# Second MLP of a three-part kernel: second product in float32r parts, low parts on GpSimd, no magnitude before the sine, another order

## The reference

```
def _moe2_ref(x, w_in, w_out) -> np.ndarray:
    h = x @ w_in
    g = h * np.cos(h)
    return (g @ w_out).astype(np.float32)
...
    attn_out = _attn_ref(**attn_kwargs)
    x = attn_out.reshape(B * S, D)
    x = _moe_ref(x=x, **moe_kwargs)
    return _moe2_ref(x=x, **moe2_kwargs)
```

## Time and profile before

| | |
|---|---|
| median of 3 runs | 2904.14 us (2903.19 to 2906.07) |
| the profiled execution, device time | 2907.74 us |
| span of the profiled execution, first to last instruction | 2905.8 us |
| PE busy | 2819.3 us (97%) |
| DVE busy | 2591.5 us (89%) |
| ACT busy | 2510.5 us (86%) |
| POOL busy | 1408.3 us (48%) |

### The profile page before, as it was taken

The page is one execution under the profiler, slowest core; times in us unless marked ns, Lnnn a source line. Parts: engine busy times, 40 slices in busy tenths (PEclk is TensorE's granted clock), DMA queues, the critical chain, the costliest instruction groups (busy, mean ns, idle before and its releaser), DMA issues.

```text
span 2905.8 us, 38889 instructions
## 1 busy us (share of the span) xinstructions
PE 2819.3 (97%) x10159; PEld 1702.5 (59%) x10159; DVE 2591.5 (89%) x3357; ACT 2510.5 (86%) x3341; POOL 1408.3 (48%) x841
## 2 busy tenths in 40 slices
PE   8969999999999999999999899999999999999999
PEld 5535555555555555555555466666666666666665
DVE  4559999999999999999999899999999999999998
ACT  4449999999999999999999788888888888888887
POOL 0019999999999999999999600000000000000000
PEclk9979999999999999999999999999999999999999
DMA  4200000000002000000000000000000000000000
GB/s 121 82 14 11 7 10 10 7 10 10 7 10 68 11 10 7 10 7 10 10 7 7 1 7 11 11 10 11 11 13 10 11 10 11 10 11 10 11 10 14
DMA packets 25713, 45.68 MB, mean 16 GB/s; under 512 B 2888, under 2 KB 11880, under 8 KB 25384
## 3 DMA queue, kind: packets, MB, share of 16 engines
q1 hardware_dynamic: 25640, 44.92, 5.1%
HBM read 16.99 MB, written 12.78 MB: 10 GB/s over the span
## 4 chain that ended last, share of the span: by engine, by line
PE 50%; POOL 32%; issue 10%; ACT 4%; DVE 3%; POOLq 1%; DMA 0%; ACTq 0%; DVEq 0%; SPq 0%
PE bank L816 24%; POOL work L304 18%; PE bank L905 18%; POOL work L302 13%; PE bank L760 2%; PE bank L740 2%; PE bank L809 1%; ACT work L380 1%; ACT work L372 1%; PE bank L733 1%; DVE work L630 1%; PE bank L896 1%; ACT work L383 1%; PE bank L750 1%; POOLq L300 1%
## 5 line engine op out<-in xcount | busy, mean ns | idle before, releaser
L816 PE MATMUL bank<-work,v 128*128 128x480 f32 x3328 | 1486.5, 569 | 21.3 <-ACT tokens_t L389 20.8
L816 PEld LDWEIGHTS bank<-work,v 128*128 128x128 f32 x3328 | 618.1, 189 | 438.6 <-issue 386.0
L809 PE MATMUL bank<-part_hi,stack_now 96*128 96x480 f32 x2496 | 695.0, 405 | 24.8 <-DVE work L630 4.5
L809 PEld LDWEIGHTS bank<-part_hi,stack_now 96*128 96x128 f32 x2496 | 424.5, 189 | 386.4 <-DVE work L630 272.1
L304 POOL TENSOR_TENSOR work<-work 128x960 f32<-128x960 f32 x278 | 625.8, 2251 | 23.2
L692 DVE SCALAR_TENSOR_TENSOR work<-work,bank 128x960 f32<-128x960 int32 x416 | 479.7, 1153 | 83.4 <-ACT work L441 81.2
L612 DVE SCALAR_TENSOR_TENSOR bank<-bank,coef_a,work 128x960 f32<-128x960 f32 x416 | 506.3, 1217 | 16.9 <-PE bank L809 13.0
L630 DVE SCALAR_TENSOR_TENSOR work<-bank,coef_a,work 128x960 f32<-128x960 f32 x416 | 502.7, 1208 | 1.6
L367 ACT ACTIVATE work<-work 128x960 f32<-128x960 f32 x416 | 418.7, 1006 | 78.9 <-POOL work L304 69.1
L701 DVE TENSOR_TENSOR work<-work,bank 128x960 f32<-128x960 f32 x416 | 476.9, 1146 | 0.3 <-ACT work L446 0.3
L905 PE MATMUL bank<-part_hi,w_hi 128*128 128x480 f32 x832 | 467.6, 562 | 4.3 <-DVE work L701 2.7
(11 more groups left out here) (81 smaller groups left out, 2005.4 us busy)
## 6 DMA issues: line engine op xcount, KB each, us to landing
x_ring<-in_x_dram SPq DMA_DIRECT2D x52, 240.0 KB, 2.9
x_group<-tokens_t SPq DMA_DIRECT2D x52, 240.0 KB, 2.2
out_dram<-work SPq DMA_DIRECT2D x52, 240.0 KB, 2.4
stack_now<-stack_next SPq DMA_DIRECT2D x8, 288.0 KB, 3.0
work<-in_moe_w_in_dram SPq DMA_DIRECT2D x1, 1024.0 KB, 10.0
w_raw<-in_moe_w_in_dram SPq DMA_DIRECT2D x1, 1024.0 KB, 5.1
v<-in_moe_w_out_dram SPq DMA_DIRECT2D x2, 0.5 KB, 10.7
ind<-in_inducing_dram SPq DMA_DIRECT2D x1, 16.0 KB, 1.8
```

What stands on the lines that cost most here:

```text
L809: mm = pe.matmul(place_out[:, t, :], stack_now[:, i, w], part_hi[0:K3, place, :], start=start, stop=stop, skip_group_check=not start)
L816: mm = pe.matmul(sums, v[:, 2 * u + t, :], g[:, t * GROUP:(t + 1) * GROUP], start=(2 * u + t == 0), stop=(2 * u + t == CHUNKS - 1))
```

## The change

The hidden values are now split at 0.25 turns off: L495 adds 0.25 before the rounding, so the remainder h - 2 pi turns lies in a range on which sine of (remainder + pi/2) can be taken directly. Both magnitude instructions (L433, L696) are gone. The product h cos(h) is written in place, into `angle`, which has four buffers instead of three, and `act2` is gone.

Three of four chunks of the second product go in float32r parts, with three matmuls each (`parts_out`, L968): ScalarE copies the product into a high part `act2_hi` (L508), GpSimd subtracts it to make the low part `act2_lo` (L361). An even unit has both of its chunks in parts (960 columns, **wide** below), an odd unit only the first (480 columns, **narrow**); its second chunk stays a float32 matmul. The weights `v2` are split by GpSimd in four pieces before the first product. The parts lie where `stack_now` was.

GpSimd also splits each group's tokens (`high_y` L344, `low_y` L349). The two output copies move from ScalarE to VectorE (L729, L735). TensorE's step k is now `end2(k)`, `begin2(k + 5)`, and a due `turn_out`; ScalarE's is L495 of unit k+4, L499 of k+3, L508 of k+2; VectorE's L749 of k+4 and L755 of k+3; GpSimd's L361 of k+2. L749 of unit n waits for `end2` of unit n-4, L508 of unit n for `end2` of unit n-2. The diff, cut to its core:

```diff
-PART_Y, KEEP_OUT_T, TURN_OUT, KEEP_OUT = -5, 11, 10, 13
+HID2, TURN2, SINE, HIGH, LOW = 5, 4, 3, 2, 2
+PART_Y, KEEP_OUT_T, TURN_OUT, KEEP_OUT = -9, 9, 11, 12
...
+        v2_hi = at(stack_at, "v2_hi", [P, CHUNKS, C], F32R)
+        act2_hi = at(stack_at + 4 * F, "act2_hi", [P, 2, UNIT], F32R)
+        act2_lo = at(stack_at + 4 * F + 8 * UNIT, "act2_lo", [P, 2, UNIT], F32R)
...
-        angle = [cut(2), cut(3), cut(4)]
-        act2 = [cut(5), cut(6), cut(7)]
+        angle = [cut(2), cut(3), cut(4), cut(5)]
...
+            def low_part(n0, k):
+                n, w = n0 + k, slice(0, split_to(k))
+                pool.wait_ge(act2_hi_ready, n + 1)
+                nc.gpsimd.tensor_tensor(act2_lo[:, k % 2, w], angle[k % 4][:, w], act2_hi[:, k % 2, w].bitcast(F32),
+                                        ALU.subtract).then_inc(act2_parted, 1)
+            def units2(n0, ks):
+                for k in ks:
+                    g = group_due(k, PART_Y)
+                    new = g is not None and exists(n0 // GROUP_UNITS + g)
+                    if new:
+                        high_y(n0 // GROUP_UNITS + g, y_place(g))
+                        pool.wait_ge(y_hi_ready, n0 // GROUP_UNITS + g + 1)
+                    if k + LOW >= 0 and exists_unit(n0 + (k + LOW)):
+                        low_part(n0, k + LOW)
+                    if new:
+                        low_y(n0 // GROUP_UNITS + g, y_place(g))
+            high_y(0, y_place(0))
+            pool.wait_ge(y_hi_ready, 1)
+            low_y(0, y_place(0))
+            pool.wait_ge(v2_loaded, 16)
+            pool.wait_ge(hid_ready, UNITS)
+            for j in range(CHUNKS // 4):
+                part_v2(j)
...
-                    nc.scalar.activation(q[:, SPLIT:], q[:, SPLIT:], ACT.Abs).then_inc(act_folded, 1)
...
-                    nc.scalar.activation(halves(turns[k % 2]), buf(k), ACT.Identity, scale=1.0 / (2 * pi)).then_inc(turns_ready, 1)
...
-                    nc.scalar.activation(q, q, ACT.Sin, scale=-1.0, bias=pi / 2).then_inc(cos_ready, 1)
...
+                    nc.scalar.activation(halves(turns[j % 2]), buf(j), ACT.Identity, scale=1.0 / (2 * pi), bias=0.25).then_inc(turns_ready, 1)
+                if k + SINE >= 0 and exists_unit(n0 + (k + SINE)):
+                    n, q = n0 + (k + SINE), angle[(k + SINE) % 4]
+                    act_.wait_ge(angle_ready, n + 1)
+                    nc.scalar.activation(q, q, ACT.Sin, bias=pi / 2).then_inc(cos_ready, 1)
+                if k + HIGH >= 0 and exists_unit(n0 + (k + HIGH)):
+                    n, j, w = n0 + (k + HIGH), k + HIGH, slice(0, split_to(k + HIGH))
+                    act_.wait_ge(act2_ready, n + 1)
+                    if not isinstance(n, int) or n >= 2:
+                        act_.wait_ge(act2_used, n - 1)
...
+                    nc.scalar.copy(act2_hi[:, j % 2, w], angle[j % 4][:, w]).then_inc(act2_hi_ready, 1)
...
-                    if later or n >= 3:
-                        dve.wait_ge(act2_ready, n - 2)
+                    if not isinstance(n, int) or n >= 4:
+                        dve.wait_ge(act2_used, n - 3)
...
+                    q = halves(angle[j % 4])
+                    dve.wait_ge(cos_ready, n + 1)
+                    nc.vector.tensor_tensor(q, q, buf(j), ALU.mult).then_inc(act2_ready, 1)
...
+                    if (t + 1) * GROUP <= split_to(k):
+                        pairs = ((v2_hi, act2_hi[:, b, w]), (v2_hi, act2_lo[:, b, w]), (v2_lo, act2_hi[:, b, w]))
+                    else:
+                        pairs = ((v2, angle[k % 4][:, w]),)
...
-                pe.wait_ge(act2_ready, n + 1)
+                pe.wait_ge(act2_parted, n + 1)
...
-                    if exists_unit(n0 + (k + LEAD)):
-                        begin2(n0, k + LEAD)
+                    if k >= 0 and exists_unit(n0 + k):
+                        end2(n0, k)
+                    if k + HID2 >= 0 and exists_unit(n0 + (k + HID2)):
+                        begin2(n0, k + HID2)
```

More of the change, by code:

```diff
@@ L316, in _, with high_y @@
             units(LAST, range(1, UNITS - LAST))
+            def high_y(g, place):
+                y = tokens_t[:, bass.ds(g * GROUP, GROUP)]
+                later = not isinstance(g, int)
+                if later or g >= PLACES:
+                    pool.wait_ge(hid2_ready, (g - PLACES + 1) * GROUP_UNITS)
+                else:
+                    pool.wait_ge(num_ready, UNITS - (PLACES - 1 - g) * GROUP_UNITS)
+                    pool.wait_ge(y_kept, g + 1)
+                nc.gpsimd.tensor_copy(part_hi[:, place, :], y).then_inc(y_hi_ready, 1)
@@ new lines, in _ @@
+            high_y(0, y_place(0))
[5 more added lines that the diff above has]
+                part_v2(j)
+            units2(0, range(PART_Y + 1, PEEL))
+            with pool.Fori(0, LOOPS // 2) as i:
+                n0 = pool.snap(i * 2 * BODY)
+                units2(n0, range(PEEL, 2 * BODY + PEEL))
+            units2(LAST, range(PEEL, UNITS - LAST))
@@ new lines, in keep_out @@
+            def keep_out(g, place):
+                dve.wait_ge(out_turned, g + 1)
+                if not isinstance(g, int) or g >= 1:
+                    dve.wait_ge(out_written, g * 16)
+                nc.vector.tensor_copy(out_sb, place[0:SUB, :]).then_inc(out_ready, 1)
+            def unit2(n0, k):
+                g = group_due(k, KEEP_OUT)
+                if g is not None and exists(n0 // GROUP_UNITS + g):
+                    keep_out(n0 // GROUP_UNITS + g, out_bank(g))
+                if k + TURN2 >= 0 and exists_unit(n0 + (k + TURN2)):
+                    n, j = n0 + (k + TURN2), k + TURN2
@@ L704, in units2 @@
                 for k in ks:
[L705 to L709 removed]
+                    unit2(n0, k)
             unit(LAST, UNITS - LAST - 1)
[L712 removed]
             keep_last_y()
             dve.wait_ge(act_ready, UNITS)
[L715 removed]
@@ L716, in _ @@
-            units2(0, range(1, PEEL))
+            units2(0, range(-TURN2, PEEL))
             with dve.Fori(0, LOOPS // 2) as i:
@@ L906, in product_in, with parts_out @@
                 return mm
+            def parts_out(sums, k):
+                u, b = k % GROUP_UNITS, k % 2
+                for t in range(2):
+                    c, w = 2 * u + t, slice(t * GROUP, (t + 1) * GROUP)
+                    if (t + 1) * GROUP <= split_to(k):
+                        pairs = ((v2_hi, act2_hi[:, b, w]), (v2_hi, act2_lo[:, b, w]), (v2_lo, act2_hi[:, b, w]))
+                    else:
+                        pairs = ((v2, angle[k % 4][:, w]),)
+                    for i, (lhs, rhs) in enumerate(pairs):
+                        mm = pe.matmul(sums, lhs[:, c, :], rhs, start=(c == 0 and i == 0), stop=(c == CHUNKS - 1 and i == len(pairs) - 1))
+                return mm
             def begin2(n0, k):
@@ L940, in steps2 @@
                         turn_out(n0 // GROUP_UNITS + g, out_bank(g))
-                    if k >= 0 and exists_unit(n0 + k):
-                        end2(n0, k)
-            steps2(0, range(-3, -2))
+            steps2(0, range(-HID2, -HID2 + 1))
             steps(LAST, range(UNITS - LAST - 2, UNITS - LAST - 1))
-            steps2(0, range(-2, -1))
+            steps2(0, range(-HID2 + 1, -HID2 + 2))
             steps(LAST, range(UNITS - LAST - 1, UNITS - LAST))
-            steps2(0, range(-1, PEEL))
+            steps2(0, range(-HID2 + 2, PEEL))
             with pe.Fori(0, LOOPS // 2) as i:
```

105 lines of the change are left out of this document (40 added, 65 removed).

## The result

The changed kernel takes **2819.5 us** (median of 4 runs, 2816.08 to 2820.59) against 2903.66 for the kernel before, run beside it (4 runs, 2903.05 to 2906.07): a ratio of 0.9707, with a 95% interval of 0.969 to 0.9723. The forecast was 2830, in a range of 2808 to 2865. The sign and the source of the gain were right. The sum is 10.5 us too high, and mostly in the very wait on which it spent most of its working. One of the ten executions of experiment 1 took 3952.67 us, at a granted clock of 0.65 where the others have 0.99, and is left out of its median.

The account below looks back on a forecast made before the run. The prediction took TensorE to bound the second MLP: 2905.8 span - 92.0 (product in parts) + 16.6 (new wait) - 1.9 (join) + 3.5 (end) = 2832.0 span, hence 2830 us median, range 2808 to 2865.

Parts of the forecast that it names:

- The product in parts: TensorE's second product: 12 of 16 chunks save 0.148 us each, 1.77 a group, -92.0 us in 52 groups.
- cost nothing by load: Second MLP: the work moved onto ScalarE, VectorE and GpSimd fits inside TensorE's group time of 22.0 us, adding nothing.
- The low part at 2.25: GpSimd's wide subtraction takes 2.25 us, the median of L304, between bounds of 1.14 and 2.53; a narrow one 1.15.
- held up: Rival: GpSimd's wide low part takes 2.53 us, the chain is 0.44 late, 2859 us; chance 0.17.
- in need of a second pass: Rival: GpSimd needs a rounding pass too, a wide low part costs 3.40 us, 2949 us, slower than before; chance 0.12.
- The new wait: Wide `end2` waits for its low part: chain 5.52 against TensorE's window 5.36, two of four stall, 0.32 a group, +16.6 us.
- the rival in which TensorE alone sets the pace: Rival: the chain through GpSimd is 0.16 or more shorter than forecast, nothing stalls, 2813 us; chance 0.20.
- the forecast's own case: Parts save TensorE time, less some stalls for the low part: 2818 to 2848 us; chance 0.48.
- Join and end: Start of the second MLP -1.9 us (token parts earlier, `begin2` of unit 3 at 1665.2); last `end2` units' waits +3.5 us.
- VectorE's margin of 0.1: From `end2`'s end VectorE's angle and product take 2.5 us against TensorE's 2.61 or more: holds by 0.1, no cost.
- The token work's 0.1 to spare: GpSimd's token copy and subtraction (1.75 us) end at about 8.5, the next high part is ready at 8.6: no cost.
- No loss by the shared ports: GpSimd beside VectorE in the second MLP: every VectorE instruction has a PSUM operand, so neither delays the other, loss nothing.

Follow-up runs that it names:

- experiment 1: The changed kernel with the second product back in plain float32 matmuls, the parts still made but unread: 2904.18 us, ratio 1.0003 to the kernel before.
- experiment 2: The changed kernel with TensorE waiting for the low part only after all matmuls that don't read it: 2816.65 us, ratio 0.9702.
- experiment 3: The changed kernel with each wide low part made in two GpSimd instructions of 480 columns: 2827.86 us, ratio 0.974.
- experiment 4: The changed kernel with each wide low part made in four GpSimd instructions of 240 columns: 2856.73 us, ratio 0.984.
- experiment 7: The changed kernel with the narrow units' high part made by VectorE instead of ScalarE, on its own semaphore: 2881.99 us, ratio 0.9913.
- experiment 9: The changed kernel with a second, long satisfied wait (for the product) ahead of GpSimd's low part: 2819.54 us, ratio 0.971.
- experiment 11: The changed kernel with the token parts of groups 1 and on made by VectorE instead of GpSimd: 2831.48 us, ratio 0.9753.
- experiment 10: All chunks in parts, low part used last, six angle buffers (2808.7 us), with token parts of groups 1 and on moved to VectorE: 2910.06 us, ratio 1.0025.
- experiment 5: The changed kernel with all 16 chunks of the second product in parts, so every unit is wide: 2861.77 us, ratio 0.9842.
- experiment 12: All chunks in parts, low part used last, six angle buffers (2808.7 us), with GpSimd's token work spread over three gaps: 2779.78 us, ratio 0.9579.

## Why the prediction was right, and where its sum was off

**The product in parts, -92.0 us: right.** The six matmuls start 0.22 apart (2213.29, 2213.51). Without stalls the period should have been 23.78 - 1.77 = 22.01; the change has 22.07 and experiment 2, without the wait, 22.03. Experiment 1 gives it all back.

**ScalarE, VectorE, GpSimd "cost nothing by load": right.** They are busy for 987, 921 and 765 of 1080 us. The copies took 0.65 to 0.68 for 0.66 and 0.70, the high part 0.98 for 1.00. Experiment 1 shows that what they were relieved of was worth nothing beside the old product.

**The low part at 2.25: right** (2.26, at most 2.28), and so GpSimd was neither held up nor in need of a second pass. The narrow one took 1.23, for 1.15: an instruction has a fixed share, which experiments 3 and 4 show, too (four of 240 columns take 2.69).

**The new wait, +16.6 us: the step that failed.** The window, the order of the chain and how close it is held, and so did the number of units that pay. Which of them pay did not: in experiment 4 a stall didn't spare the next wide unit, because of the token work. One borrowed term was too large, the 0.26 until GpSimd starts. It was read from L302 in the first MLP and taken for a price of waiting on another engine. Measured are 0.08 behind ScalarE, 0.09 behind VectorE (experiment 7), 0.08 with a second wait (experiment 9). With 0.08 and a high part of 0.98 the chain is 5.33 against a window of 5.36, and the stalls come to 0.04 (experiment 2) to 0.06 a group (22.07 against 22.01), 2 to 3 us. That is the rival in which TensorE alone sets the pace, by the reason named for it, "GpSimd starts sooner behind ScalarE". It had 0.20, and the forecast's own case 0.48. Its 2813 rests on a span of 2815.4, and the span is 2816.6; the rest of its distance is the step from span to median, below. That the time also fell into the forecast's own 2818 to 2848 is luck: without that step's 4.6 us it would have been 2815. At such an edge a lateness of 0.16 became 16.6 us, and the 0.26 had one kind of row behind it, from another loop.

**Join and end, +1.6 us:** the two together came to -0.2 (89.2 less 89.0). `begin2` of unit 3 came at 1662.79, not at 1665.2, and the wait ahead of the last `end2` units was 0.60 + 1.97 = 2.6 us instead of 3.8. These two readings are 2.4 and 1.2 us better than forecast, where the sum is better by 1.8 only; how the 0.2 is split between join and end isn't measured.

**From span to median.** The forecast took 1.66 off the span. In the changed kernel the profiled run's device time is 1.83 above its span and 1.07 below the median, so 2.9 come on top. Altogether 2830.3 - 13.6 (stalls) - 1.8 (join, end) + 4.6 = 2819.5.

**VectorE's margin of 0.1: held.** In the steady stretch the weight loads of `begin2` never waited over 0.4 for it, and its matmuls are in no row of waits. Experiments 7 and 11 put 0.4 us into every other unit and 1.1 once a group, and lost 62 and 12 us.

**The token work's 0.1 to spare: held, barely.** In the change the subtraction ends at 2221.69 and the next wide low part starts at 2221.73, 0.08 behind its high part. Experiment 4 shows what happens when it doesn't fit.

**No loss by the shared ports: right**, for the reason given: every steady VectorE instruction has a PSUM operand. Experiment 10, in a kernel with a fuller GpSimd, takes that condition away and pays 101 us.

What stays open is why L302 starts 0.26 behind its releaser. It isn't the releasing engine. A second wait cost nothing at the wide low part and 0.06 behind GpSimd's own copy, so waits may be a part of it; its third wait, its scalar operands and its register work weren't tried.

## What to carry to other kernels

When a helper engine feeds TensorE, compare the whole chain from its release to its result with what TensorE has between, not the helper's load: TensorE waited for a GpSimd that was 87% busy in one order (experiment 5), and not for one that was 94% busy in another (experiment 12). Let TensorE first use what is ready first, and put the helper's side work in pieces behind several units; here these two and two more buffers took a kernel from 42 us behind the change (experiment 5) to 40 us ahead of it. Take a start latency from the same kind of instruction with the same kind of waits, and where chain and window differ by less than that borrowed term, give the case without stalls at least an equal chance.

## What the runs showed of the hardware

- GpSimd starts 0.08 to 0.09 us behind the end of the instruction that releases it, whether ScalarE or VectorE; L302's 0.26 is an exception whose cause is open. Behind its own copy, with a wait for it, it starts 0.16 later, and 0.22 with a second wait in between.
- A two-input GpSimd instruction with a float32r output takes what the float32 one does: 2.25 us for 128 x 960 (the earlier trace rows and L361). 480 columns take 1.23 and 240 about 0.70.
- VectorE's copy from SBUF to SBUF, 0.40 us alone, took 2.22 when it was issued 0.3 us into a GpSimd instruction of 2.27, and its subtraction with two SBUF inputs made the GpSimd instruction that started beside it 0.39 longer.
- Behind 13 of 45 gaps of up to 1.9 us TensorE's next matmuls ran at the 1.2 GHz level; the mean granted clock of that kernel's stretch is 0.98, where the others have 1.00. An estimate of its price: 13 times half of 3.3 us in 45 groups is 0.5 a group, so about 25 of the 101 us of experiment 10 are the clock, given up by a wait that VectorE caused.
